# Attention loop of a three-stage kernel: its place in the instruction stream, its start-up products and two of its waits are changed

## The reference

```python
def reference(q, k, v, mem_k, mem_v, moe, moe2):
    # 1. chunked attention: 4 batches, 8 heads, 768 tokens, head size 64
    for c in range(24):                       # chunks of 32 queries
        # 16 keys to the left, the chunk, 8 to the right, and 8 memory keys
        a = softmax(q_c @ k_full.T / 8)
        out[:, :, chunk] = a @ v_full
    x = rows of out                           # (3072, 512)
    # 2. each token goes to one of 8 experts, 384 tokens each, greedily by logit
    logits = x @ w_gate
    for e in range(8):
        out[mask] = relu(x[mask] @ w1[e]) @ w2[e]
    # 3. h = x @ w_in; u = h * softmax(h); layer norm of u times g_ln; then @ w_out
```

## Time and profile before

| what | us |
|---|---|
| median of 3 runs | 745.43 |
| the profiled execution | 741.89 |
| its span, first to last instruction | 740.2 |
| PE busy | 697.8 (94%) |
| DVE, ACT, POOL busy | 526.6, 328.1, 321.2 |
| mean granted TensorE clock | 0.963 of full |

### The profile page before, as it was taken

How to read it: one execution, slowest core, us unless ns; L and a number is a source line. 1 busy time by engine, 2 the same in 40 slices (tenths; PEclk the granted TensorE clock), 3 DMA queues, 4 the chain that set the end, 5 groups by cost and what they waited for, 6 DMA issues and landing times.

```text
span 740.2 us, 18070 instructions
## 1 busy us (share of the span) xinstructions
PE 697.8 (94%) x7190; PEld 622.9 (84%) x7190; DVE 526.6 (71%) x1937; ACT 328.1 (44%) x540; POOL 321.2 (43%) x242
## 2 busy tenths in 40 slices
PE   7999963899999999999999999999999999999992
PEld 5899952698899889988998899889988998999881
DVE  4677776787888788878887887788778877451240
ACT  1455536332581257135713571357135713571360
POOL 2111127881772277227722762276227622762011
PEclk8999975799999999999999999999999999999997
DMA  8999993601330233023302330233023302330001
GB/s 313 357 384 382 386 390 126 213 8 58 101 114 30 60 111 115 30 64 108 115 29 71 101 114 30 71 101 114 30 75 98 114 29 73 115 99 30 0 15 43
DMA packets 24925, 89.09 MB, mean 120 GB/s; under 512 B 3360, under 2 KB 3360, under 8 KB 24864
## 3 DMA queue, kind: packets, MB, share of 16 engines
q0 software_dynamic: 13056, 46.14, 19.2%
q1 hardware_dynamic: 11808, 42.17, 15.0%
HBM read 75.71 MB, written 12.58 MB: 119 GB/s over the span
## 4 chain that ended last, share of the span: by engine, by line
PE 93%; DVE 3%; issue 1%; ACT 0%; POOL 0%; DVEq 0%; POOLq 0%; ACTq 0%
PE banks L604 26%; PE banks L606 24%; PE banks L605 24%; PE banks L511 3%; PE banks L633 3%; PE banks L490 3%; PE banks L461 3%; PE bank L472 2%; PE bank L502 2%; PE banks L617 1%; PE bank L597 1%; PE bank L531 1%; PE bank L538 1%; DVE hot_b L1149 0%; DVE xl L1335 0%
## 5 line engine op out<-in xcount | busy, mean ns | idle before, releaser
L1489 POOL TENSOR_TENSOR wl<-raw,wh 128x1024 fp32r<-128x1024 f32 x60 | 146.4, 2440 | 30.7 <-ACT wh L834 29.6
L1483 POOL DMA_INDIRECT raw<-w,w_idx x60 | 67.2, 1121 | 147.7 <-DVE w_idx L1199 110.6
L604 PE MATMUL banks<-xh,wh 128*128 128x384 f32 x256 | 90.7, 354 | 2.1 <-DVE xl L1335 2.1
L604 PE MATMUL banks<-hh,wh 128*128 128x384 f32 x256 | 90.3, 353 | 0.0
L606 PE MATMUL banks<-xh,wl 128*128 128x384 f32 x256 | 86.5, 338 | 0.0
L605 PE MATMUL banks<-xl,wh 128*128 128x384 f32 x256 | 86.3, 337 | 0.0
L606 PE MATMUL banks<-hh,wl 128*128 128x384 f32 x256 | 86.3, 337 | 0.0
L605 PE MATMUL banks<-hl,wh 128*128 128x384 f32 x256 | 85.9, 335 | 0.0
L604 PE MATMUL banks<-wout_h,uh 128*128 128x512 f32 x192 | 79.1, 412 | 0.0
L604 PE MATMUL banks<-win_h,yh 128*128 128x512 f32 x192 | 77.5, 403 | 0.0
L606 PE MATMUL banks<-wout_h,ul 128*128 128x512 f32 x192 | 75.4, 393 | 0.0
(11 more groups left out here) (212 smaller groups left out, 1564.3 us busy)
## 6 DMA issues: line engine op xcount, KB each, us to landing
unit<-qk_in SPq DMA_DIRECT2D x24, 768.0 KB, 6.2
vr<-v_in SPq DMA_DIRECT2D x24, 520.0 KB, 4.9
x_rows<-x_keep SPq DMA_DIRECT2D x20, 256.0 KB, 5.5
prep_early<-w_in SPq DMA_DIRECT2D x2, 512.0 KB, 8.0
x_rows<-x_sb SPq DMA_DIRECT2D x4, 256.0 KB, 5.2
prep_first<-w_in SPq DMA_DIRECT2D x2, 512.0 KB, 6.3
prep_first<-w_out SPq DMA_DIRECT2D x2, 512.0 KB, 7.8
prep_rest<-w_out SPq DMA_DIRECT2D x2, 512.0 KB, 9.3
```

What stands on the lines that cost most here:

```text
L604: nc.tensor.matmul(bank, stat_h, mov_h, start=first, stop=False)
L1483: gp.indirect_dma_start(stage(s, c), None, table, bass.IndirectOffsetOnAxis(ap=w_idx[:, c % WCH:c % WCH + 1], axis=0))\
L1489: gp.tensor_tensor(wl[:, c % WCH, :], stage(s, c), wh[:, c % WCH, :].bitcast(F32), ALU.subtract)\
```

## The change

- The loop of PE is opened with an argument (`head_slot`) that places its first instruction at slot 0 of a block of 256 instruction slots; the slots ahead of it are branched over.
- In the first of the four steps of each iteration, PE waits between `scores` and `probs_T` until the scores just issued are done, and ahead of `gate` for `small_in`. The wait for `small_in` ahead of the loop is gone.
- The three blank products of 128x512 become ten of 32x64.
- DVE clears in another order, `pT` in two halves, and both `xT` clearings raise the semaphore by two. The two clearings of `vr` go to GpSimd, behind the identity matrix and ahead of the other constants.

```diff
-WARM = 3
+WARM = 10
...
                 if not known or i < NT:
                     scores(i, r, n)
+                if not known and r == 0:
+                    pe.wait_ge(scores_ps, i + 1)
                 if not known or i <= NT:
                     probs_T(i, (r - 1) % DEEP)
+                if not known and r == 0:
+                    pe.wait_ge(small_in, 32)
                 gate(i, (r - 3) % DEEP)
...
             for _ in range(WARM):
-                nc.tensor.matmul(PT_PS[:, :], blank[:, 0:P], blank, start=True, stop=True)
+                nc.tensor.matmul(PT_PS[0:CHUNK, 0:D], blank[:, 0:CHUNK], blank[:, 0:D], start=True, stop=True)
             pe.wait_ge(consts, 1)
-            pe.wait_ge(small_in, 32)
-            with pe.Fori(0, NT // DEEP) as b:
+            with nc.Fori(0, NT // DEEP, 1, engines=[pe.engine], head_slot={pe.engine: 0}) as b:
...
             nc.vector.memset(pr[:, 1, :, :, :], 0.0).then_inc(probs, 1)
-            nc.vector.memset(xT[:, 1, :, :], 0.0).then_inc(xT_sb, 1)
             nc.vector.memset(x_sb[:, 1, :, :, :], 0.0).then_inc(x_ready, 1)
-            nc.vector.memset(pT[:, :, :, :], 0.0).then_inc(pT_sb, BLANK_PT)
-            nc.vector.memset(vr[:, RING - 2 * CPT:RING - CPT, :, :], 0.0).then_inc(v_loaded[DEEP - 2], 16)
-            nc.vector.memset(xT[:, 0, :, :], 0.0).then_inc(xT_sb, BLANK_XT - 1)
+            nc.vector.memset(pT[:, 0, :, :], 0.0).then_inc(pT_sb, 1)
+            nc.vector.memset(xT[:, 1, :, :], 0.0).then_inc(xT_sb, BLANK_XT // 2)
             nc.vector.memset(x_sb[:, 2, :, :, :], 0.0).then_inc(x_ready, 1)
-            nc.vector.memset(vr[:, RING - CPT:RING, :, :], 0.0).then_inc(v_loaded[DEEP - 1], 16)
+            nc.vector.memset(pT[:, 1, :, :], 0.0).then_inc(pT_sb, 1)
+            nc.vector.memset(xT[:, 0, :, :], 0.0).then_inc(xT_sb, BLANK_XT // 2)
             nc.vector.memset(x_sb[:, 3, :, :, :], 0.0).then_inc(x_ready, 1)
...
+            for i in (DEEP - 2, DEEP - 1):
+                gp.memset(vr[:, CPT * i:CPT * i + CPT, :, :], 0.0).then_inc(v_loaded[i], 16)
             gp.memset(ones_b[:, :], 1.0)
```

## The result

The changed kernel takes 747.38 us (median of 20 runs), the kernel before, on the same chip and in turn with it, 743.36 us (20 runs). The ratio is 1.0047 (95% interval 1.0032 to 1.0062): 3.5 us slower by the ratio (the two medians lie 4.0 apart), where the forecast said 4.3 faster. The profiled execution took 748.08 us with a span of 746.3, against 741.89 and 740.2 before. These two lie 6.2 us apart, since the one of before was a quick one of its kind; the traces tell where the time went, the ratio how much of it is there on average.

A forecast was written before the change was run, and what follows sets the result against it. PE, busy 94% of the span, was taken as the bound, with code fetch setting the first iteration's pace. Terms -5.0 + 1.25 - 0.6 gave -4.3 us: median 745.4 becomes 741.1, range 738.4 to 745.2.

The forecast's parts named there:

- The pauses, read as code: PE's pauses of 2.30 and 0.28 us in the first iteration stand on borders of 256-instruction code blocks, fetched late.
- Blanks, clearing, gate weights, transfers: Start-up: blanks end and transposes start at 3.8 us, scores at 5.3; clearing hidden, gate weights and transfers cost nothing.
- Term 1: First iteration: with code blocks 4.0 us apart, the fifth step begins at 21.15 instead of 26.15, -5.0 us.
- its own upper end: First iteration: at 5.6 us for each code block, the fifth step begins at 27.5, no gain.
- terms 2 and 3: The wait for own scores in five iterations, +1.25 us, and the pause in the last value products going, -0.58 us.
- The clock: First iteration: 6.5 us at clock 0.50 would hide code behind slow products; fifth step at 21.7, nearly the same.
- Code comes late, or the clock drops: Rival, first iteration: first block takes 5.6 us, later ones nearer 4.3; fifth step about 23, net -2.5, 742.9; chance 0.22.
- Slower: the loop no longer fits: Rival, every iteration: a block falls out and is fetched anew, five pauses of 2.3 us, +7, 752.6; chance 0.05.
- The branches back: Loop end: by the skill's rule each of five branches back would pause for a fetch; the sum left this out.

The follow-up runs named there:

- run with slot 128: The kernel before with only the loop's head placed at slot 128 of the block shared with the start-up code; ratio 1.0036 to the kernel before.
- changed, no own wait: The changed kernel without PE's wait for the scores it has just issued; ratio 1.0051 to the kernel before.
- before, data paced: The kernel before with its first eleven unit transfers each issued once the one two places before had landed; ratio 1.0008.
- the four paced kernels: Unit transfers paced in the changed kernel (1.001), the kernel before (1.0008), and the six-blank kernel with two (0.9967) or three (1.0003) under way.
- six blanks, paced by two: Changed kernel without placement and own-scores wait, six small blanks, first eight unit transfers each issued once the one two before landed; 742.1 us, ratio 0.9967.

## Why the prediction was wrong

**The pauses, read as code: right.** They stand on borders 256 instructions apart, and the borders moved to 256, 512, 768 and 1024 as computed: three pauses inside scores. The run with slot 128 paused after 384 instructions, as it had to.

**Blanks, clearing, gate weights, transfers: right in time, wrong in clock.** Scores of the first unit began at 5.9 (forecast 5.3) against 8.2 before. What I missed: the first transposes took 1.05 us where they took 0.44 before, so they ran at half pace. PE had then been at work for 2.3 us, before for 5.4. The whole first step took 1.1 us more than a full-pace step, its pause left out.

**Term 1, "26.15 to 21.15, -5.0", is the step that failed.** It was +4.8 in the profile. It had "the four blocks behind it come at 3.0 + 4.0 = 7.0, 11.0, 15.0 and 19.0". They came at 7.5, 14.2, 22.9 and in time for 28. Three things were wrong in it. I took 4.0 us for a block as if it were a property of the chip, from readings that ran from 3.7 to 5.6, and chose near the low end, though the one reading from the time in question was 5.6. An earlier start moves the requests into the stretch in which the DMA engines are full of unit data; there three blocks took 5.2, 6.7 and 8.7 us from being asked for (2.3 to 7.47, 7.47 to 14.18, 14.18 to 22.86). And I did not compare what the placement changes in itself: before, 175 of the loop's instructions came with the start-up block and three blocks had to be fetched; from slot 0 it is four. The text had both numbers (175 and the four times) and never set one against the other. The placement alone costs 0.67%, and taking it out of the change gives the loss back. And the prediction passed over its own upper end: "with 5.6 it is 27.5 and no gain" is 1.4 us later than before, which with terms 2 and 3 makes 747.4. No chance was put on it. That this meets the measured 747.38 is in part luck, since the blocks were not evenly late and term 2 was too high.

**The clock.** "Should the clock stand at 0.50 for 6.5 us again" was priced at nearly nothing. It stood there for 20.4 us. How the fifth step comes about can be added up from the chains: the start of the first transposes, 13.68 us for four steps at full pace, the pauses, and a rest, which is work at less than full pace.

| profiled execution | first transposes | pauses | rest | fifth step |
|---|---|---|---|---|
| before | 7.05 | 2.58 | 2.84 | 26.15 |
| changed | 3.96 | 6.04 | 7.29 | 30.97 |
| changed, no own wait | 3.96 | 7.26 | 5.14 | 30.04 |
| before, data paced | 7.08 | 3.43 | 0.70 | 24.89 |

So of the 4.8 us, -3.1 are the earlier start, +3.5 the pauses and +4.4 the slow pace. The low clock did not wait for the long pauses: in the changed kernel it began at 9.2, behind a pause of 0.78 us, and the pauses of 2.15 and 3.11 came later. What sets it off stays open. Nor is its share in this pair of executions the usual one. Each execution has a mean granted clock on record: 0.954 and 0.963 for the two profiled ones, but on average 0.957 over the 20 of the changed kernel and 0.958 over the 119 of the kernel before in the experiments. At the same mean clock of 0.959 the changed kernel takes 746.65 us (median of 7), the kernel before 743.87 (median of 20). These were not run in turn, so the 2.8 us between them are rough, but they say that most of the measured 3.5 us is not the clock's.

**Term 2, +1.25, was mis-sized.** The wait costs 0.14 us an iteration, +0.7. The release came 0.04 us behind the last product, and the transposes' own time lengthened by 0.07.

**Term 3, -0.58: right**, -0.5 in the trace.

**The rivals.** "Code comes late, or the clock drops" had the mechanism but was priced at one block of 5.6, and net -2.5: the same low figure. "Slower: the loop no longer fits" did not happen: no code moved between the fetches at the start and 103 us, so the loop's blocks stayed. The slower outcome came by a way for which I had no rival, the extra block in the first iteration.

**The branches back.** The rule of the Trainium skill ("Runtime: NRT & Kernel Launch", "Instruction fetch mechanics") that a taken branch out of a window of two pages forces a fetch: the trace of after does not agree either, with five branches back and no code transfer from 29.5 to 102.9 us. The same section's blocks of 256 instructions agree with every border seen here.

## What to carry to other kernels

Count how many blocks of 256 instructions the first pass of a loop has to fetch, and let the loop's head share the block of the start-up code if that saves one; aligning a head to a block's start can cost more than it tidies. A code block is a DMA transfer like the others, and a start at which all data is issued at once can make the first pass wait for its own instructions. Before moving a start forward it is worth trying to pace the data to what is needed next, and measuring each pacing: of the four paced kernels here one was faster (0.9967) and three were as before. And a duration that was read where a queue was short does not hold where it is full.

## What the runs showed of the hardware that was not expected

- A 16 KB code transfer started 1.1 us behind its request with almost no unit data queued (22.86 in the changed kernel) and 6.3 us behind it with 1.8 MB queued (14.18); its own movement took 0.9 to 1.1 us either way, and where PE waited the first instruction followed 2.3 to 2.4 us behind the start.
- More queued data does not add to it in step: 1.4 MB and 2.5 MB gave 3.5 and 3.6 us in the kernel before, and 3.3 MB gave 4.4 in the changed one, less than the 6.3 with 1.8 MB.
- The first transposes took 1.05 us when PE had been at work for 2.3 us (the changed kernel) and 0.44 when it had been for 5.4 (before), though the view by stretch gives a granted clock of 1.00 for both: that column does not show the pace at the very start.
- The low clock at the start lasted from 6.8 us (before) to 20.4 us (changed), and the length of a pause did not decide it: it came behind pauses of 0.78 us (changed) and 0.96 us (six blanks, paced by two), and not in the paced kernel of before, with pauses of 1.38, 0.52 and 1.53 us.
